# Seven block products for eight in the second phase's up product, two token tiles interleaved

## The chip, the cores and the metric

The kernel runs on one core of a Trainium2 chip. The metric is the device time of one execution in microseconds (us). Arithmetic is fp32 throughout: each fp32 operand of the large products is split into a high part, rounded to the type fp32r, and a low part, the remainder, and a product is three matmuls (high by high, high by low, low by high).

## The reference

Three layers follow each other: a retention layer with a decaying state (4 batches, 8 heads, 768 positions, head size 64), a feed-forward layer of 512 to 2048 to 512, and a second one of 512 to 1024 to 512. The last one is what the change touches. There are 3072 tokens.

```python
def _moe2_ref(x, w_in, w_out, g_ln):
    h = x @ w_in                                    # 3072 x 512 by 512 x 1024
    h_max = np.max(h, axis=-1, keepdims=True)
    e = np.exp(h - h_max)
    sm = e / (np.sum(e, axis=-1, keepdims=True) + 1e-09)
    solu = h * sm
    mu = np.mean(solu, axis=-1, keepdims=True)
    var = np.mean((solu - mu) ** 2, axis=-1, keepdims=True)
    ln = (solu - mu) / np.sqrt(var + 1e-06) * g_ln
    return (ln @ w_out).astype(np.float32)
```

## The kernel before

**Two phases.** The first phase computes retention and the first feed-forward layer in six blocks of 512 tokens and stores its result, transposed, to DRAM (x2T, stored by SP from the tile y). The second phase takes x2T in pairs of tiles of 128 tokens, 12 pairs and 24 tiles. Each engine has its own queue and runs it in program order; all order between engines is by semaphores written by hand.

**First phase, where it touches the change.** In each of 16 steps f of a block TensorE does `up(blk, f)` (12 matmuls of 512 columns) and `down(blk, f - 2)` (12 matmuls). VectorE clamps h (L610), ScalarE squares (L481), VectorE takes the maximum (L615), ScalarE copies the high part of g (L429), POOL subtracts for the low part (L670). In the last block `prepare(f)` of ScalarE and VectorE splits the second phase's w_in, its first two pairs of x2 and w_out between these steps, and POOL makes the low parts of w_out (L677). Its last two down products run behind the first up of the second phase. `evacuate`, which empties the accumulator banks to y for the last store of x2T, is called late, from the second phase's loops (ScalarE L429, VectorE L573). SP's queue holds the last four stores of x2T ahead of all its work of the second phase.

**Second phase.** `up(t)` is 24 matmuls: x's high and low parts are the stationary operand (128 x 128), w_in the moving one (512 columns), two banks of 512 columns for a tile, four of the eight banks for two tiles. VectorE searches the maximum over 1024 in PSUM (L866), ScalarE takes the exponential with its sum (L816), VectorE multiplies e, 1/sum and h from PSUM with the sum of the result (L878, "softening"), ScalarE squares with a sum (L821), POOL raises the variance to the power -0.5 (L924), VectorE normalises to z (L889) and transposes within squares of 32 (L893). SP stores z to DRAM and reads it back in four parts so that it comes back transposed. ScalarE copies its high part (L794) and VectorE subtracts for the low part (L861), in two halves. `down(t)` is 24 matmuls with z as the stationary operand into one of two banks; it waits for the output of two tiles ahead to be copied out (`o_ready`). ScalarE copies the result (`output`, L794) and SP stores it.

The order on TensorE is up 0, the last two downs of the first phase, up 1, up 2, and from then on up t with down t - 3 behind it, so a tile's z has some three tiles of TensorE's work to come back; the last downs follow without ups. The two split operations of x for a later pair (ScalarE L794, VectorE L853) stand ahead of the maximum of every other tile. A load of x2T for pair n waits for the end of up of pair n - 2.

Of the kernel before, what the change touches and what calls it, by code (L numbers as in the profile page):

```python
# [11 lines left out]
P = 128  # L12
# [8 lines left out]
KT = DM // P  # L21
# [35 lines left out]
def passes(a, b):  # L57
# [3 lines left out]
STATISTICS = ("h_max", "neg_max", "e_sum", "e_sum_eps", "e_inv", "s_sum", "neg_mean", "sq_sum", "var",  # L61
              "rstd")


def place(nc):
# [38 lines left out]
    split("x", [P, KT, BLK])  # L104
    plain("y", [P, KT, BLK])
# [23 lines left out]
    split_in_place("x2_0", [P, KT, 2 * P])  # L129
# [3 lines left out]
    split_in_place("x2_1", [P, KT, 2 * P])  # L133
    assert cursor[0] <= w_at + 5 * 8192
    for name in ("e", "solu", "dev", "z"):
        plain(name, [P, FF2])
    plain("o", [P, 2, DM])
    plain("zq", [P, 2, P // SQ, FT2, SQ])
    plain("zt", [P, 2, P // SQ, FT2, SQ])
    for n in range(LAG2):  # L140
        split(f"zT{n}", [P, FT2, P])
    assert cursor[0] <= w_at + 13 * 8192
# [3 lines left out]
def first_phase(nc, block, io, sem, mem, x2_dram, finish):  # L146
# [9 lines left out]
    with ExitStack() as ctx:  # L156
# [38 lines left out]
        def _(sp):  # L195
# [74 lines left out]
            for m in range(KT):  # L270
                sp.wait_ge(sem["x2_stored"][m], 16)
            x2_view = x2_dram.rearrange("(kt p) t -> p kt t", p=P)
            sp.dma_start(mem["x2_0_raw"][:, :, :], x2_view[:, :, 0:2 * P]).then_inc(sem["x2_loaded"][0], 16)
# [4 lines left out]
            sp.dma_start(mem["x2_1_raw"][:, :, :], x2_view[:, :, 2 * P:4 * P])\  # L278
                .then_inc(sem["x2_loaded"][1], 16)
# [147 lines left out]
        def _(act):  # L427
# [28 lines left out]
            def prepare(f):  # L456
                if 5 <= f < 5 + KT:
                    kt = f - 5
                    act.wait_ge(sem["w2_in_loaded"][kt], 16)
                    copy(mem["w2_in"][0][:, kt, :], mem["w2_in_raw"][:, kt, :]).then_inc(sem["w2_in_hi"], 1)  # L460
                elif f == 9:
                    act.wait_ge(sem["x2_loaded"][0], 16)
                    copy(mem["x2_0"][0][:, :, :], mem["x2_0_raw"][:, :, :]).then_inc(sem["x2_hi"], 1)
# [5 lines left out]
                elif f == 15:  # L469
                    act.wait_ge(sem["x2_loaded"][1], 16)  # L470
                    copy(mem["x2_1"][0][:, :, :], mem["x2_1_raw"][:, :, :]).then_inc(sem["x2_hi"], 1)
# [33 lines left out]
        def _(dve):  # L505
# [69 lines left out]
            def prepare(f):  # L575
                if 5 <= f < 5 + KT:
                    kt = f - 5
                    dve.wait_ge(sem["w2_in_hi"], kt + 1)
                    tt(mem["w2_in"][1][:, kt, :], mem["w2_in_raw"][:, kt, :],
                       mem["w2_in"][0][:, kt, :].bitcast(F32), ALU.subtract).then_inc(sem["w2_in_lo"], 1)  # L580
                elif f == 9:
                    dve.wait_ge(sem["x2_hi"], 1)
                    tt(mem["x2_0"][1][:, :, :], mem["x2_0_raw"][:, :, :],
                       mem["x2_0"][0][:, :, :].bitcast(F32), ALU.subtract).then_inc(sem["x2_lo"], 1)
# [8 lines left out]
                elif f == 15:  # L593
                    dve.wait_ge(sem["x2_hi"], 2)
                    tt(mem["x2_1"][1][:, :, :], mem["x2_1_raw"][:, :, :],
                       mem["x2_1"][0][:, :, :].bitcast(F32), ALU.subtract).then_inc(sem["x2_lo"], 1)
# [38 lines left out]
        def _(pool):  # L635
# [28 lines left out]
            def dense(blk):  # L664
                for f in range(FT1):
# [8 lines left out]
                    if blk == BLOCKS - 1 and 12 <= f < FT1:  # L674
                        for piece in (2 * (f - 12), 2 * (f - 12) + 1):
                            pool.wait_ge(sem["w2_out_hi"], piece + 1)
# [14 lines left out]
def second_phase(nc, block, io, sem, mem, x2_dram, z_dram, finish):  # L691

    TILES = TOKENS // P
    SEGS = [slice(n * 512, (n + 1) * 512) for n in range(FF2 // 512)]
    x2_view = x2_dram.rearrange("(kt p) t -> p kt t", p=P)
# [311 lines left out]
```

## Time and profile before

| | us |
|---|---|
| median of 3 runs | 880.04 (879.76 to 880.24) |
| the profiled execution, its time | 879.7 |
| its span, first to last instruction | 877.6 |
| TensorE busy | 871.1 (99%) |
| VectorE busy | 407.8 (46%) |
| ScalarE busy | 284.0 (32%) |
| POOL busy | 206.0 (23%) |

Busy time is the time in which an engine had an instruction in work. The page also cuts the span in 40 slices. TensorE's granted clock is full in all of them; in the 12 slices of the second phase VectorE is at 4 to 7 tenths, ScalarE at 2 to 4, and DMA engines at about 4 tenths. Matmuls overlap, so one of 512 columns has a duration of 0.39 us though they start every 0.227. A group of instructions is named by its line, engine, operation, and what it writes and reads.

### The profile page before, as it was taken

What the parts mean: (1) busy time and instruction counts of PE and PEld (TensorE: products, weight loads), DVE (VectorE), ACT (ScalarE), POOL (GpSimd) and SP (SyncE); (2) the same over time, 40 slices, a digit from 0 to 9 for tenths busy, and PEclk for the clock granted to TensorE, in tenths of its full rate; (3) what the DMA queues carried; (4) which work ended last, traced back from release to release, by engine and by line L of the source; (5) the groups of instructions that cost most, each with busy time, mean ns of one, the idle gap of its engine ahead of it and who ended that gap; (6) DMA issues with size and microseconds to landing.
All of it is one profiled execution on the core that took longest, in us unless ns stands there. A gap on an engine that the chain in (4) does not pass through costs nothing.

```text
span 877.6 us, 11925 instructions
## 1 busy us (share of the span) xinstructions
PE 871.1 (99%) x4888; PEld 712.7 (81%) x4888; DVE 407.8 (46%) x645; ACT 284.0 (32%) x454; POOL 206.0 (23%) x186
## 2 busy tenths in 40 slices
PE   8999999999999999999999999999999999999998
PEld 7788878888878888888878888888888888888886
DVE  5555443334332343323433332443666666666672
ACT  3333342212221132212321232334334444444442
POOL 2645532232223222232221122226000000000000
PEclk9999999999999999999999999999999999999999
DMA  9921111111111102111111004300444444444433
GB/s 338 375 68 49 49 49 49 49 52 46 61 49 49 57 28 96 49 49 37 49 37 49 25 1 167 121 1 1 144 133 156 156 144 144 144 155 147 150 125 132
DMA packets 50742, 82.85 MB, mean 94 GB/s; under 512 B 5248, under 2 KB 23680, under 8 KB 50688
## 3 DMA queue, kind: packets, MB, share of 16 engines
q1 hardware_dynamic: 50688, 82.08, 27.8%
q8 instruction: 39, 0.64, 0.3%
q14 instruction: 15, 0.12, 0.0%
HBM read 56.90 MB, written 25.17 MB: 94 GB/s over the span
## 4 chain that ended last, share of the span: by engine, by line
PE 94%; DVE 2%; DMA 2%; ACT 1%; POOL 1%; SPq 1%; issue 0%; DVEq 0%; POOLq 0%; ACTq 0%
PE acc L390 30%; PE h L360 29%; PE o_ps L778 14%; PE h L763 12%; PE att L297 2%; PE att L308 2%; PE att L332 1%; PE att L322 1%; DMA q<-in_q 1%; DMA x_raw<-x2T 0%; PE acc L308 0%; POOL w_out_lo L677 0%; DMA z<-zq 0%; PE h L377 0%; SPq L197 0%
## 5 line engine op out<-in xcount | busy, mean ns | idle before, releaser
L390 PE MATMUL acc<-g_hi,w 128*128 128x512 f32 x768 | 257.3, 396 | 0.0
L360 PE MATMUL h<-x_hi,w 128*128 128x512 f32 x760 | 250.0, 390 | 0.5 <-DVE x_lo L565 0.5
L670 POOL TENSOR_TENSOR g_lo<-g_raw,g_hi 128x512 fp32r<-128x512 f32 x96 | 123.4, 1286 | 399.7 <-ACT g_hi L429 399.7
L481 ACT ACTIVATE g_raw<-g_raw,half_bias 128x512 f32<-128x512 f32 x96 | 69.5, 724 | 337.9 <-DVE g_raw L610 337.9
L390 PEld LDWEIGHTS acc<-g_hi,w 128*128 128x128 f32 x768 | 144.2, 188 | 35.0 <-issue 3.4
L360 PEld LDWEIGHTS h<-x_hi,w 128*128 128x128 f32 x760 | 142.7, 188 | 30.6 <-DVE x_lo L565 0.9
L610 DVE TENSOR_SCALAR g_raw<-h 128x512 f32<-128x512 f32 x96 | 66.3, 691 | 180.7 <-PE acc L390 179.9
L390 PE MATMUL acc<-g_lo,w 128*128 128x512 f32 x384 | 149.7, 390 | 0.0
L360 PE MATMUL h<-x_lo,w 128*128 128x512 f32 x380 | 148.0, 389 | 0.0
L615 DVE TENSOR_TENSOR g_raw<-h,g_raw 128x512 f32<-128x512 f32 x96 | 66.4, 692 | 70.0 <-ACT g_raw L481 70.0
L429 ACT ACTIVATE g_hi<-g_raw 128x512 fp32r<-128x512 f32 x96 | 60.7, 632 | 72.7 <-DVE g_raw L615 72.7
L390 PEld LDWEIGHTS acc<-g_lo,w 128*128 128x128 f32 x384 | 72.2, 188 | 14.0
L360 PEld LDWEIGHTS h<-x_lo,w 128*128 128x128 f32 x380 | 71.4, 188 | 14.6
L763 PE MATMUL h<-w_in_hi,x_hi 128*128 128x512 f32 x192 | 74.8, 390 | 0.0
L763 PE MATMUL h<-w_in_lo,x_hi 128*128 128x512 f32 x192 | 74.7, 389 | 0.0
L778 PE MATMUL o_ps<-w_out_lo,zT_hi 128*128 128x512 f32 x192 | 74.7, 389 | 0.0
L763 PE MATMUL h<-w_in_hi,x_lo 128*128 128x512 f32 x192 | 74.7, 389 | 0.0
L778 PE MATMUL o_ps<-w_out_hi,zT_hi 128*128 128x512 f32 x192 | 74.7, 389 | 0.0
L778 PE MATMUL o_ps<-w_out_hi,zT_lo 128*128 128x512 f32 x192 | 74.7, 389 | 0.0
L924 POOL TENSOR_TENSOR rstd<-var,power 128x1 f32<-128x1 f32 x24 | 13.2, 548 | 227.5 <-DVE var L886 227.5
L816 ACT ACTIVATE e<-h,neg_max 128x1024 f32<-128x1024 f32 x24 | 26.8, 1117 | 86.7 <-DVE neg_max L868 86.6
L821 ACT ACTIVATE dev<-solu,neg_mean 128x1024 f32<-128x1024 f32 x24 | 27.7, 1153 | 46.8 <-DVE neg_mean L881 46.8
(76 smaller groups left out, 842.0 us busy)
## 6 DMA issues: line engine op xcount, KB each, us to landing
z<-zq SPq DMA_DIRECT2D x24, 512.0 KB, 2.7
zt<-z SPq DMA_DIRECT2D x96, 128.0 KB, 2.9
kT<-in_kT SPq DMA_DIRECT2D x24, 256.0 KB, 2.6
q<-in_q SPq DMA_DIRECT2D x24, 256.0 KB, 2.6
v<-in_v SPq DMA_DIRECT2D x24, 256.0 KB, 2.9
x2T<-y SPq DMA_DIRECT2D x24, 256.0 KB, 2.6
x_raw<-x2T SPq DMA_DIRECT2D x12, 512.0 KB, 4.3
out<-o SPq DMA_DIRECT2D x24, 256.0 KB, 2.1
```

Source lines behind the costliest of these rows:

```text
L297: last = mm(out[e][:, p * P:(p + 1) * P], kT[half(e), p, :], q[half(e), p, :], start=True, stop=True)
L360: last = mm(hb[f % 2][:, :], ww, xx[:, kt, :], start=kt == 0 and t == 0, stop=kt == KT - 1 and t == 2)
L390: last = mm(acc[m][:, :], ww, gg[:, f % 2, :], start=f == 0 and t == 0, stop=f == FT1 - 1 and t == 2)
L429: return nc.scalar.activation(out, in_, ACT.Copy)
L481: nc.scalar.activation(gate[:, f % 2, :], gate[:, f % 2, :], ACT.Square, bias=half_bias[:, 0:1], scale=0.5).then_inc(sem["squared"], 1)
L610: nc.vector.tensor_scalar(gate[:, f % 2, :], h, 1.0, -1.0, ALU.min, ALU.max)\
L615: tt(gate[:, f % 2, :], h, gate[:, f % 2, :], ALU.max).then_inc(sem["gmax"], 1)
L670: tt(g[1][:, f % 2, :], gate[:, f % 2, :], g[0][:, f % 2, :].bitcast(F32), ALU.subtract)\
L763: last = mm(hp[t % 2][:, seg], xx[:, kt, cols], ww[:, kt, seg], start=kt == 0 and i == 0, stop=kt == KT - 1 and i == 2)
L778: last = mm(op[t % 2][:, :], zz[:, f, :], ww[:, f, :], start=f == 0 and i == 0, stop=f == FT2 - 1 and i == 2)
L816: nc.scalar.activation(e[:, :], hp[t % 2][:, :], ACT.Exp, bias=st("neg_max", t), accum_out=st("e_sum", t)).then_inc(sem["e_ready"], 1)
L821: nc.scalar.activation(dev[:, :], solu[:, :], ACT.Square, bias=st("neg_mean", t), accum_out=st("sq_sum", t)).then_inc(sem["sq_sum"], 1)
```

## The change

The up product of a pair of tiles is a product of 256 x 512 by 512 x 1024. As 2 x 2 blocks by 2 x 2 blocks (token tile by half of the inner dimension; half of the inner dimension by half of the columns) it is done with seven block products for eight (Strassen's scheme in Winograd's form). A block product is 128 x 256 by 256 x 512, that is two steps by three passes, 6 matmuls. The sums that it needs are made once for w_in (VectorE, during the last block of the first phase, three sums of 128x1024, split in high and low parts as well) and for each pair for x (POOL, `sums_of_x2`: four operations over 256 elements, in a row through semaphores), and split by ScalarE and VectorE. VectorE's `join(n)` adds the block products together to h in SBUF, and four of its additions also give the maximum. The splits of the next pair stand within the join, from pair 1 on. All seven blocks pass through six banks (`pb`), of which for pair 0 only the first three or four are used, because the accumulators of the first phase still hold two others.

The two tiles of a pair then go side by side through maximum, exponential and so on, second tile first. z is made by ScalarE (`normalize`, an activation with rstd as scale and a bias) from a bias that VectorE computes. e and squares share a tile; h is read from SBUF. The downs go by slots s, two per pair. The order of TensorE is up 0, the last two downs of the first phase, up 1, down 0, up 2, down 1, down 2, up 3, down 3, down 4, and so on to up 9, down 15, down 16, up 10, down 17, up 11, downs 18 to 23.

The core of the diff:

```diff
@@ first phase, SP
+            for n in range(2):
+                sp.wait_ge(sem["g_used"], FT1 * (BLOCKS - 1) + 8 + 2 * n)
+                sp.dma_start(mem[f"x2_{n}_raw"][:, :, :], x2_view[:, :, n * 2 * P:(n + 1) * 2 * P])\
+                    .then_inc(sem["x2_loaded"][n], 16)
             store_x2(BLOCKS - 1)
@@ POOL
+            def sums_of_x2(n):
+                raw, out = mem[f"x2_{n % 2}_raw"], mem[f"x2_sum{n % 2}_raw"]
+                first, second = slice(0, P), slice(P, 2 * P)
+                pool.wait_ge(sem["x2_loaded"][n % 2], 16 * (n // 2 + 1))
+                tt(out[:, 0, :, :], raw[:, 0:2, second], raw[:, 2:4, second], ALU.add)\
+                    .then_inc(sem["x2_summed"], 1)
+                tt(out[:, 2, :, :], raw[:, 0:2, first], raw[:, 0:2, second], ALU.subtract)\
+                    .then_inc(sem["x2_summed"], 1)
...
@@ second phase, TensorE
-                for seg in SEGS:
-                    for kt in range(KT):
-                        for i, (xx, ww) in enumerate(passes(x[t // 2 % 2], w_in)):
-                            last = mm(hp[t % 2][:, seg], xx[:, kt, cols], ww[:, kt, seg],
-                                      start=kt == 0 and i == 0, stop=kt == KT - 1 and i == 2)
+                product(pb[0], a(0, FIRST), b(0, LEFT))
+                wait(pe, sem["h_max"], 2 * n)
+                product(pb[1], a(1, FIRST), b(1, LEFT))
+                if n == 0:
+                    pe.wait_ge(sem["gmax"], BLOCKS * FT1)
+                product(pb[2], s(1), t(1))
+                product(pb[3], s(2), b(0, RIGHT))
+                if n == 0:
+                    pe.wait_ge(sem["part_copied"], 1)
+                if n == 1:
+                    for par in range(2):
+                        pe.wait_ge(sem["acc_free"][par], 2 * BLOCKS)
+                product(bank4(n), a(1, SECOND), t(2))
+                pe.wait_ge(sem["taken"], 5 * n + 1)
+                product(bank5(n), s(0), t(0))
+                if n == 0:
+                    pe.wait_ge(sem["taken"], 2)
+                product(bank3(n), s(3), b(1, RIGHT))
...
+            for n in range(PAIRS2 - 1):
+                up(n)
+                if n == 0:
+                    finish["down"]()
+                if n >= 2:
+                    down(2 * n - 3)
+                if 1 <= n < PAIRS2 - 2:
+                    down(2 * n - 2)
+            up(PAIRS2 - 1)
+            for s in range(TILES - 6, TILES):
+                down(s)
@@ second phase, ScalarE
+            for n in range(PAIRS2):
+                copy_part(n)
+                if 1 <= n < PAIRS2 - 1:
+                    split_x(n + 1)
+                if n:
+                    split_z(2 * n - 2)
+                exponential(n, SECOND)
+                exponential(n, FIRST)
+                if n:
+                    split_z(2 * n - 1)
+                squares(n, SECOND)
+                squares(n, FIRST)
+                normalize(n, SECOND)
+                normalize(n, FIRST)
+                if n == 0:
                     finish["act_evacuate"]()
+                if 2 <= n < PAIRS2 - 1:
+                    output(2 * n - 3)
+                if 1 <= n < PAIRS2 - 2:
+                    output(2 * n - 2)
+            for s in range(TILES - 6, TILES - 4):
+                output(s)
@@ second phase, VectorE
+            def join(n):
+                dve.wait_ge(sem["part_copied"], n + 1)
+                dve.wait_ge(sem["products"], 7 * n + 2)
+                add_with_maximum(h2[:, FIRST, LEFT], pb[1][:, :], part[:, :], -3.4e38, st("h_first", FIRST))\
+                    .then_inc(sem["taken"], 1)
+                dve.wait_ge(sem["products"], 7 * n + 3)
+                tt(part[:, :], pb[2][:, :], part[:, :], ALU.add).then_inc(sem["taken"], 1)
+                if 1 <= n < PAIRS2 - 1:
+                    split_x(n + 1, False)
+                dve.wait_ge(sem["products"], 7 * n + 4)
+                dve.wait_ge(sem["taken"], 5 * n + 2)
+                tt(part7[:, :], pb[3][:, :], part[:, :], ALU.add).then_inc(sem["taken"], 1)
+                if 1 <= n < PAIRS2 - 1:
+                    split_x(n + 1, True)
...
+            for n in range(PAIRS2):
+                join(n)
+                if n:
+                    split_z(2 * n - 2)
+                soften(n, SECOND)
+                soften(n, FIRST)
+                if n:
+                    split_z(2 * n - 1)
+                if n == 0:
                     finish["dve_evacuate"]()
+                variance(n, SECOND)
+                variance(n, FIRST)
+                bias(n, SECOND)
+                bias(n, FIRST)
+                turn_squares(n, SECOND)
+                turn_squares(n, FIRST)
@@ second phase, SP
+            sp.wait_ge(sem["g_used"], BLOCKS * FT1)
+            for n in range(PAIRS2):
+                if n + 2 < PAIRS2:
+                    load_x2(n + 2)
+                if 2 <= n < PAIRS2 - 1:
+                    store(2 * n - 3)
+                put_z(2 * n)
+                put_z(2 * n + 1)
+                get_z(2 * n)
+                get_z(2 * n + 1)
+                if 1 <= n < PAIRS2 - 1:
+                    store(2 * n - 2)
```

## Rows read from the trace of the kernel before

**Rows 1.** The page, busy time of each engine and share of the span
```profile
PE 871.1 (99%) x4888; PEld 712.7 (81%) x4888; DVE 407.8 (46%) x645; ACT 284.0 (32%) x454; POOL 206.0 (23%) x186
```

**Rows 2.** Chain that ended last, in order of time: start, us, what
```profile
624.28 3.24 DMA z<-zq
...
629.47 4.11 DMA x_raw<-x2T
...
645.97 5.44 PE o_ps L778 x24
...
847.25 27.21 PE o_ps L778 x120
874.48 0.60 ACT o L794
```

**Rows 3.** Groups by line, 620 to 860 us: busy us, mean ns
```profile
L893 DVE STREAM_TRANSPOSE zq<-z 128x1024 f32<-128x1024 f32 x24 | 29.9, 1246 | 0.8
L878 DVE SCALAR_TENSOR_TENSOR solu<-e,e_inv,h 128x1024 f32<-128x1024 f32 x23 | 29.4, 1280 | 0.8
L861 DVE TENSOR_TENSOR zT_lo<-zt,zT_hi 128x512 fp32r<-128x512 f32 x45 | 28.3, 667 | 1.8 <-ACT zT_hi L794 1.8
L866 DVE TENSOR_REDUCE h_max<-h 128x1 f32<-128x1024 f32 x23 | 28.0, 1216 | 0.0
...
L816 ACT ACTIVATE e<-h,neg_max 128x1024 f32<-128x1024 f32 x23 | 25.7, 1117 | 81.3 <-DVE neg_max L868 81.2
L889 DVE TENSOR_SCALAR z<-solu,neg_mean,rstd 128x1024 f32<-128x1024 f32 x24 | 19.5, 813 | 16.0 <-POOL rstd L924 16.0
...
L853 DVE TENSOR_TENSOR x_lo<-x_raw,x_hi 128x1024 fp32r<-128x1024 f32 x10 | 12.2, 1220 | 0.9 <-ACT x_hi L794 0.9
L794 ACT ACTIVATE o<-o_ps 128x512 f32<-128x512 f32 x20 | 11.5, 577 | 0.0
```

**Rows 4.** Timeline of VectorE at the transition: start, us, operation, idle before
```profile
609.14 0.69 DVE L615 TENSOR_TENSOR g_raw<-h,g_raw 128x512 f32<-128x512 f32 x1 [0.79 <-ACT g_raw L481]
611.48 1.47 DVE L595 TENSOR_TENSOR x_lo<-x_raw,x_hi 128x1024 fp32r<-128x1024 f32 x1 [1.65 <-ACT x_hi L429]
615.41 1.23 DVE L866 TENSOR_REDUCE h_max<-h 128x1 f32<-128x1024 f32 x1 [2.46 <-POOL power L920]
```

**Rows 5.** Timeline of all engines, 742 to 747 us, a tile's statistics
```profile
742.71 0.15 DVE L873 TENSOR_SCALAR e_sum_eps<-e_sum 128x1 f32<-128x1 f32 x1 [1.27 <-ACT e L816]
...
744.60 1.15 ACT L821 ACTIVATE dev<-solu,neg_mean 128x1024 f32<-128x1024 f32 x1 [1.93 <-DVE neg_mean L881]
...
745.88 0.15 DVE L886 TENSOR_SCALAR var<-sq_sum 128x1 f32<-128x1 f32 x1 [1.31 <-ACT dev L821]
...
746.69 0.81 DVE L889 TENSOR_SCALAR z<-solu,neg_mean,rstd 128x1024 f32<-128x1024 f32 x1 [0.66 <-POOL rstd L924]
```

**Rows 6.** Timeline of POOL, two subtractions of 512 elements each
```profile
600.95 2.54 POOL L677 TENSOR_TENSOR w_out_lo<-w_out_raw,w_out_hi 128x512 fp32r<-128x512 f32 x2
...
611.83 3.51 POOL L677 TENSOR_TENSOR w_out_lo<-w_out_raw,w_out_hi 128x512 fp32r<-128x512 f32 x2
```

**Rows 7.** Timeline of SP's queue at the transition
```profile
621.75 1.79 SPq L222 DMA_DIRECT2D x2T<-y  x4
...
627.54 1.75 SPq L731 DMA_DIRECT2D zt<-z  x4
```

**Rows 8.** The page, DMA issues: count, KB each, us to landing
```profile
z<-zq SPq DMA_DIRECT2D x24, 512.0 KB, 2.7
```

**Rows 9.** Timeline of ScalarE, the first z that comes back
```profile
631.95 1.15 ACT L794 ACTIVATE zT_hi<-zt 128x512 fp32r<-128x512 f32 x2 [1.99 <-DMA zt<-z]
```

**Rows 10.** Timeline of TensorE at the start of the kernel
```profile
1.19 2.93 PE L411 MATMUL acc<-warm 128*128 128x256 f32 x6 [1.19 <-DVE warm L621]
...
7.29 1.56 PE L411 MATMUL acc<-warm 128*128 128x256 f32 x6
```

**Rows 11.** Windows: busy of five engines, granted clock, DMA share, GB/s
```profile
0.00:5.00 5.00, 3.74 (x18) 2.69 (x20) 0.28 (x2) 1.49 (x2) 0.20 (x4) 1.00 0.59 200
```

More of the change, by code:

```diff
@@ L141, in place @@
         split(f"zT{n}", [P, FT2, P])
-    assert cursor[0] <= w_at + 13 * 8192
+    assert cursor[0] <= y_at
+    cursor[0] = y_at
+    plain("o", [P, 2, DM])
     return mem
@@ L742, in _ @@
+            for n in range(PAIRS2):
[9 more added lines that the diff above has]
+                    store(2 * n - 2)
+            for s in range(TILES - 5, TILES):
+                store(s)
             for par in range(2):
@@ L747, in _, with product, up, a @@
             mm = nc.tensor.matmul
-            def up(t):
-                if t == 0:
+            def product(out, a, b):
+                for k in range(2):
+                    for i, (aa, bb) in enumerate(passes([part(k) for part in a], [part(k) for part in b])):
+                        last = mm(out[:, :], aa, bb, start=k == 0 and i == 0, stop=k == 1 and i == 2)
+                last.then_inc(sem["products"], 1)
+            def up(n):
+                def a(half_k, tile):
+                    return [lambda k, x=x: x[:, 2 * half_k + k, tile * P:(tile + 1) * P]
+                            for x in mem[f"x2_{n % 2}"]]
+                def s(i):
+                    return [lambda k, x=x: x[:, i, k, :] for x in mem[f"x2_sum{n % 2}"]]
+                def b(half_k, cols):
+                    return [lambda k, w=w: w[:, 2 * half_k + k, cols] for w in w_in]
+                def t(i):
+                    return [lambda k, w=w: w[:, i, k, :] for w in w_sum]
+                if n == 0:
                     pe.wait_ge(sem["probs"], 2 * CHUNKS)
@@ L803, in split_z @@
+            def split_z(s):
+                act.wait_ge(sem["zt_loaded"][s % 2], 64 * (s // 2 + 1))
+                wait(act, sem["o_done"], s - LAG2 + 1)
                 for n in range(2):
                     fs = slice(4 * n, 4 * n + 4)
[L805 to L811 removed]
@@ L838, in _, with output @@
-            split_z(TILES - 3)
-            squares(TILES - 1)
-            output(TILES - 5)
+                    copy(zT[s % LAG2][0][:, fs, :].rearrange("p f (i c) -> p f i c", c=SQ),
+                         zt[:, s % 2, :, fs, :].rearrange("p i f c -> p f i c")).then_inc(sem["zT_hi"], 1)
+            def output(s):
+                act.wait_ge(sem["o_done"], s + 1)
+                wait(act, sem["o_stored"][s % 2], 16 * (s // 2))
+                if s == 0:
+                    for m in range(KT):
+                        act.wait_ge(sem["x2_stored"][m], 16 * BLOCKS)
+                copy(o[:, s % 2, :], op[s % 2][:, :]).then_inc(sem["o_ready"], 1)
@@ L843, in _ @@
             split_z(TILES - 1)
-            for t in range(TILES - 3, TILES):
-                output(t)
+            for s in range(TILES - 3, TILES):
+                output(s)
         @block.vector
```

404 lines of the change are left out of this document (222 added, 182 removed).

## The prediction

> **What bounds the kernel now.** I read the page's busy line first: TensorE is busy for 871.1 us of a span of 877.6 [rows 1], so only its work and its gaps count. Next the chain that ended last, in order of time: in the second phase it is groups of 24 matmuls of 5.44 us one behind the other, a tile's up product or its down product, so 0.2267 us a matmul, and the last of them ends at 874.48, 3.1 us ahead of the end [rows 2]. There is no pause that a shorter stream could move into. The other engines have room: the groups by line give what each operation costs [rows 3]. The change takes matmuls away and lengthens the chain from an up product to the z that the down product needs. The question is whether that chain, so far three tiles ahead of TensorE, stays hidden.
>
> **What goes.** A pair of tiles took 48 up matmuls and takes 7 x 6 = 42. Twelve pairs save 72 x 0.2267 = 16.3 us if TensorE never waits. Bound: no row shows another pace for this shape, so 16.3 is the whole gain.
>
> **What the other engines do for a pair, and the steady state.** VectorE loses two searches for the maximum (1.216) and two z (0.813) and gets, per pair, three additions from PSUM (0.69, [rows 4]), four additions with a maximum, and one more split of 128x1024 (1.22). The addition with a maximum is in no row; it lies between the plain PSUM addition, 0.69, and the softening operation over 1024, 1.28 [rows 3]; I take 0.75, nearest to the same shape with one small accumulator read more. Join: 4 x 0.75 + 3 x 0.69 + 2 x 1.22 + 0.3 = 7.8. The rest: z splits 2.5, softening 2 x 1.85, four small statistics 0.6, two transposes 2.5. Waits that remain: the variance to what uses rstd is 0.81 for one tile, from 745.88 to 746.69 [rows 5] and POOL and ScalarE in front of the first transpose add as much again, together 1.6. Sum 18.7 us. TensorE has 42 + 48 = 90 matmuls, 20.4 us, per pair. So VectorE goes from loosely used to 92%, yet TensorE still bounds. ScalarE gets two normalisations of 128x1024 (the nearest rows are the exponential, 1.12, and the square, 1.15 [rows 3, 5]; 1.1 taken), a copy of 0.58 and a split near 1.1; it has about 12.5 of 20.4. The new POOL sums are four operations of 256 elements. A POOL subtraction of 512 elements took 1.27 alone and 3.51 for two beside VectorE [rows 6]; in proportion 0.65 for 256, at most 1.3; I take 0.7, 2.8 per pair, off the path in the steady state. The z round trip of one pair (softening to z back in SBUF) is 18 to 19 us, and the down product wants it 25.8 us behind the end of its up product. Price of the steady state: 0.
>
> **End of the first phase.** The extra splits give VectorE at most 1 us more than an iteration's 5.44 in three iterations running, and its results lead TensorE by 3; nothing, at most 0.5.
>
> **Transition, first places.** The up product of pair 0 uses only four banks, so its sixth block waits for VectorE's first addition. VectorE waits for POOL's constant behind w_out pieces, as now: its first operation of the phase starts at 615.41 [rows 4]. Plus 0.75, the sixth block starts at 616.2; without waits it would be at 614.2, and a copy behind ScalarE's splits has used 0.2 of that. Cost 2.05. Up ends at 619.0, the two remaining down products of the first phase end at 624.4, the first four blocks of pair 1 at 629.85. The fifth block needs the accumulator banks evacuated. ScalarE does that now behind normalisation. In the trace's time: second tile's negative maximum 619.9, first tile's 620.8; exponentials, for which VectorE waits 1.27 [rows 5]; two softenings of 1.85 each, from the first small statistic at 742.71 to ScalarE's square at 744.60 [rows 5], end at 624.95; squares and variance 626.3; rstd for both and bias 627.65; normalisations to 629.4; evacuation 630.0 and 630.5. The fifth block waits 0.7. Up 1 ends at 634.65.
>
> **Transition, the long pause.** Down 0 follows here, where it used to come behind four tiles' ups. Several things now stand in series. SP's queue holds the four stores of x2T (0.45 each, [rows 7]) ahead of all else of the second phase; they wait for the late evacuation, so they end at 631.85. Behind them SP issues the load of pair 2. A load of this kind took 4.11 and a z store beside x2T stores 3.24 where 2.7 is usual [rows 2, 8]; I take 4.4: 636.25. POOL's sums wait for it: 639.0. VectorE stands inside the join of pair 1, after its second addition, since both splits of pair 2 wait for the sums. Queued behind that wait are two splits, one plain addition, the sums of the other blocks and the maxima, 2.44 + 2.25 + 1.4 + 0.3 = 6.4 to 645.4, and only then the low half of z, 0.67 for its first half: 646.2 with the passing of semaphores. z itself is back earlier: its store goes behind the load at 632.2, 3.3 later the four reads, 4.4 later [rows 7, 9] 639.9. TensorE waits from 634.65 to 646.2, 11.55. Bounds: if the additions run end to end and the sums take 0.65, 2 less; if the sums take 1.3 each, 2.4 more.
>
> **TensorE after the pause.** At the start, its first six matmuls of 256 columns took 2.93 us and the same six later 1.56, with a granted clock of 1.00 (2.4 GHz) in the row of that stretch [rows 10, 11]. So a start from idle has cost 1.37 here. I add 1.4 for the 11.5 us pause, between 0 and twice that. TensorE: Matmul & The Clock Gate, section Part 1 of the Trainium skill, says that an idle TensorE falls to 1.2 GHz and returns once busy. The matmul durations agree with it, the granted clock of the row does not; by the granted clock alone the forecast would be 1.4 lower.
>
> **The end.** Only one down product stands between up 10 and up 11, and the output of down 18 is queued on ScalarE behind the whole last pair. Count from the end of up 10: first exponential 0.95; softenings end 6.75, z halves 7.95, bias 8.8, normalised 10.1, transposed 11.4. SP has the store of output 17 in front: z store at 12.2, reads at 14.9, z back at 19.3. ScalarE is in order, so the exponential of pair 11 starts behind z's high half at 20.5 although its maximum is long there; normalised twice at 29.9, output 18 at 30.5. Down 20 wants that bank at 5.44 + 9.52 + 10.88 = 25.84. Cost 4.7. Then four downs and the same last 3.1 us.
>
> **Sum.** -16.3 + 2.05 + 0.7 + 11.55 + 1.4 + 4.7 = +4.1. The profiled execution of 879.7 (span 877.6, 2.1 around it) becomes 883.8. It lies 0.34 under the median 880.04 of the runs, so the forecast is 884.1.
>
> **Rivals.**
> *The low bounds hold together*: additions and sums 2 less, the load 0.3, no cost behind the pause 1.4, the end 1. That is 4.7 less, 879.4, within what can be told from none. For it: neighbours without a wait overlap by some 0.08 in the trace. Against: most steps here wait for the one before. Chance 0.17.
> *Faster*: the pause ends when z is back, not with the sums. It decides at whether pair 2's load leaves SP before about 627; then down 0 starts at 640.5, 5.7 earlier, and with no cost behind a shorter pause 1.4 more goes: 877.0. The order of SP's queue in the diff speaks against it, and that the evacuation stands behind the normalisations. Chance 0.12.
> *The softening slows.* It read PSUM and SBUF at 1.28 [rows 3]; now both inputs are in SBUF. The splits also read two SBUF tensors and take 1.22 for 1024, which speaks against a slower pace, but they write no accumulator. At half the pace it is 1.07 more each: 2.1 in the transition, twice 2.1 at the end, and VectorE's loop of 18.7 becomes 20.8, 0.4 over TensorE's, some 1 to 2 in total: 892. Chance 0.13. Vector Engine (DVE) Microarchitecture Reference, Points that are easy to get wrong, in the Trainium skill, says that this operation with two sources in SBUF that aren't bf16 halves its throughput. By that, 892 is the forecast; no row of the trace has that form.
> *POOL and VectorE hold each other up.* A split took 1.47 beside POOL [rows 4] and 1.22 otherwise, POOL 3.51 for two. If the sums fall on the transposes and splits, 0.25 to 1 per pair comes on a loop with 1.7 to spare; with the transition's own splits and pieces, 3 more in all: 887. Chance 0.13.
>
> **How the numbers follow.** The forecast with its own bounds (881.8 to 887) has 0.45. Faster by over 0.2% (below 878.3) is the second rival, 0.12; within 0.2%, about what a measurement of this kernel can tell from no change, is the first, 0.17; slower is the rest, 0.71. The range takes in the faster rival and the halved softening: 877 to 892.5.
>
> **What would show it.** Right: no waits of TensorE between up 3 and up 9; one pause of 10 to 13 us in front of the first down product, released by VectorE's low half of z; SP's x2T stores near 630 and the pair's load behind them; a second pause near 4.7 in front of the down product of slot 20, released by ScalarE's output. 72 matmuls fewer at 0.2267. Softening at 1.28. Wrong: a pause below 8 us, a wait of TensorE in each pair, a softening near 2.3, or an addition with maximum above 1.0.

## The result

| | us |
|---|---|
| before, median of 6 runs | 880.14 (879.76 to 882.25) |
| changed, median of 6 runs | 888.6 (886.47 to 891.81) |
| ratio changed to before | 1.0098, 95% interval 1.0076 to 1.0119 |
| profiled execution of the changed kernel, its time and span | 891.81, 890.0 |

The change makes the kernel 8.5 us slower. The forecast was 4.1 slower. The profiled execution is the longest of the six, 3.2 us over the median, which matters when its rows are added up below.

The page of the changed kernel, the line that answers to [rows 1], and its line of TensorE's granted clock in 40 slices:

```profile
PE 864.4 (97%) x4816; PEld 704.5 (79%) x4816; DVE 447.4 (50%) x772; ACT 333.1 (37%) x505; POOL 242.5 (27%) x234
...
PEclk9999999999999999999999999999979999999989
```

TensorE has 6.7 us less busy time than before where 16.3 of work went, and of the 40 slices one shows a granted clock of 7 tenths and one of 8, all others 9 or more. The chain that ended last, in order of time (start, us, what), answers to [rows 2]:

```profile
618.86 4.56 PE p L842 x12
623.42 5.48 PE acc L401 x24
...
650.85 8.28 PE o_ps L895 x24
659.14 9.52 PE p L842 x42
668.66 10.88 PE o_ps L895 x48
...
862.01 24.86 PE o_ps L895 x96
886.90 0.60 ACT o L914
```

In the steady state an up of a pair is 42 matmuls in 9.52 us and two downs are 10.88, with no wait between them from 659.14 until the sixth block of the last pair at 844. But 12 matmuls of the up of pair 0 took 4.56 where 2.72 is the pace, the 24 of the first down 8.28 instead of 5.44, and the last 96 took 24.86 instead of 21.76. The timeline of TensorE has the waits in front of them (start, us, operation, idle before and what ended it), here the sixth block of pair 0's up:

```profile
618.86 0.79 PE L842 MATMUL p<-w_sum_hi,x_sum_hi 128*128 128x512 f32 x1 [2.19 <-DVE h_first L993]
```

the first down:

```profile
650.85 0.79 PE L895 MATMUL o_ps<-w_out_hi,zT_hi 128*128 128x512 f32 x1 [11.93 <-DVE zT_lo L1077]
```

and the down of slot 20:

```profile
862.01 0.80 PE L895 MATMUL o_ps<-w_out_hi,zT_hi 128*128 128x512 f32 x1 [3.72 <-ACT o L914]
```

And the windows of these stretches (busy of five engines, then granted clock, DMA share, GB/s):

```profile
618.86:622.00 3.14, 3.14 (x7) 2.48 (x8) 2.11 (x5) 0.00 (x0) 1.80 (x2) 0.50 0.00 0
638.90:650.80 11.90, 0.02 (x1) 0.00 (x0) 6.50 (x14) 4.86 (x7) 2.85 (x4) 0.66 0.80 252
650.80:656.00 5.20, 5.15 (x12) 4.08 (x13) 4.99 (x13) 4.07 (x7) 0.00 (x0) 0.50 0.00 0
862.00:868.00 6.00, 5.99 (x14) 4.75 (x15) 0.76 (x1) 0.44 (x1) 0.00 (x0) 0.50 0.77 279
```

After each of the three longer pauses the granted clock is 0.50, that is 1.2 GHz, for 3.3, 5.4 and 6.0 us, and matmuls of 512 columns start every 0.43 us (618.86 to 622.0 holds seven).

**The account of this execution**, from start times of matmuls less 0.2267 for the one before: TensorE stood still for 0.52 (ahead of the up of pair 0), 2.34, 0.36, 12.09, 0.46 (sixth block of the last pair) and 3.88 us, 19.65 in all. The slow stretches cost 1.68 + 2.68 + 2.93 = 7.29. The second phase was reached 1.72 later than in the trace of before. In the first 20 us of this execution the granted clock was 0.91, with 0.50 from 7.8 to 11.2 us. The 1.72 belongs to the execution and not to the change: the same point of the first phase comes 0.55 later than in before in e4's profiled execution, and 3.2 later in e6's. -16.32 + 19.65 + 7.29 + 1.72 = 12.34; measured between the last matmuls' ends (886.90 and 874.48) 12.42.

### The profile page after: what moved, and what is told of

The parts are those of the page before. It is cut to its first block, busy times and chain, and to the rows that moved or that the text cites. A ratio compares the mean times of both kernels' runs of the same rounds, so it can differ in the third digit from the quotient of the medians.

```text
span 890.0 us, 12101 instructions
## 1 busy us (share of the span) xinstructions
PE 864.4 (97%) x4816; PEld 704.5 (79%) x4816; DVE 447.4 (50%) x772; ACT 333.1 (37%) x505; POOL 242.5 (27%) x234
## 4 chain that ended last, share of the span: by engine, by line
PE 90%; DVE 3%; DMA 2%; POOL 2%; issue 1%; ACT 1%; SPq 0%; DVEq 0%; ACTq 0%; POOLq 0%
PE acc L401 30%; PE h L371 28%; PE o_ps L895 14%; PE p L842 10%; PE att L308 3%; PE att L319 2%; PE att L343 1%; PE att L333 1%; POOL w_out_lo L720 1%; DVE solu L1047 1%; DMA q<-in_q 1%; DVE h L993 1%; DMA x_raw<-x2T 1%; DVE zT_lo L1077 0%; ACT solu L941 0%
## 5 line engine op out<-in xcount | busy, mean ns | idle before, releaser
L895 PE MATMUL o_ps<-w_out_hi,zT_hi 128*128 128x512 f32 x192 | 77.3, 403 | 15.7 <-DVE zT_lo L1077 11.9
L895 PE MATMUL o_ps<-w_out_lo,zT_hi 128*128 128x512 f32 x192 | 76.8, 400 | 0.0
L895 PE MATMUL o_ps<-w_out_hi,zT_lo 128*128 128x512 f32 x192 | 76.6, 399 | 0.0
L895 PEld LDWEIGHTS o_ps<-w_out_hi,zT_hi 128*128 128x128 f32 x192 | 37.4, 195 | 24.3 <-DVE zT_lo L1077 12.4
L914 ACT ACTIVATE zT_hi<-zt 128x512 fp32r<-128x512 f32 x48 | 27.5, 620 | 56.4 <-DMA zt<-z 56.4
L895 PEld LDWEIGHTS o_ps<-w_out_hi,zT_lo 128*128 128x128 f32 x192 | 37.3, 194 | 8.1
L895 PEld LDWEIGHTS o_ps<-w_out_lo,zT_hi 128*128 128x128 f32 x192 | 37.4, 195 | 7.9
L532 DVE TENSOR_TENSOR pr<-att,mask 128x512 f32<-128x512 f32 x40 | 25.7, 685 | 25.2 <-PE att L308 25.2
```

Source lines behind the costliest of these rows:

```text
L532: tt(of("pr", c)[:, e, :, :], by_pair(s_banks(c)[e]), mask[:, e, :, :], ALU.mult)\
L895: last = mm(op[s % 2][:, :], zz[:, f, :], ww[:, f, :], start=f == 0 and i == 0, stop=f == FT2 - 1 and i == 2)
L914: return nc.scalar.activation(out, in_, ACT.Copy)
```

## The experiments

All were run beside the kernel before, whose medians in the three groups of runs were 880.49, 880.09 and 880.62. Theory A is mostly the forecast's chain, with TensorE's clock added as what it under-counted. The changed kernel was not run again beside them, so the gains below are against its 888.6, whose own six runs spread over 5.3 us. Its ratio's interval, 1.0076 to 1.0119, overlaps those of e3, e5 and e9 and touches e1's: by time alone these four gains are not clear of noise, and what they show is in their traces. Gains and losses of the others are clear.

| run | edit to the changed kernel | median us | ratio to before, 95% |
|---|---|---|---|
| e1_fill | unread matmuls in two pauses | 885.45 | 1.0064 (1.0052 to 1.0076) |
| e2_load_first | load of pair 2 ahead of x2T stores | 883.41 | 1.0033 (1.0020 to 1.0046) |
| e3_pool_last | w_out pieces 4, 5 behind the constant | 886.37 | 1.0069 (1.0057 to 1.0082) |
| e4_output | output 18 ahead of the last squares | 883.65 | 1.0039 (1.0027 to 1.0051) |
| e5_evac | evacuation ahead of normalisations | 887.66 | 1.0082 (1.0068 to 1.0096) |
| e6_three | e2, e3 and e4 | 876.72 | 0.9957 (0.9944 to 0.9971) |
| e7_filled | e6, z store first, output 20 earlier, fill | 874.52 | 0.9940 (0.9925 to 0.9955) |
| e8_double | first block product twice | 900.99 | 1.0236 (1.0222 to 1.0250) |
| e9_pool_clear | POOL's pieces behind the splits | 886.49 | 1.0070 (1.0057 to 1.0082) |
| e10_best | e7 with e9's edit and x2T stores behind z's reads | 872.32 | 0.9907 (0.9892 to 0.9923) |

### e1_fill: is it the clock?

```diff
+                if s == 0:
+                    pe.wait_ge(sem["w2_out_lo"], 1)
+                    fill(op[1], 50)
+                if s == TILES - 4:
+                    pe.wait_ge(sem["h_max"], 2 * PAIRS2)
+                    fill(pb[0], 16)
                 wait(pe, sem["o_ready"], s - 1)
```

> Edit: 50 matmuls of 512 columns whose results nobody reads are put ahead of the first down product, and 16 ahead of the down product of slot 20, so that TensorE works through most of its two long pauses (12.0 and 3.9 us); the waits stay. Theory A (what the forecast missed is the clock after a pause): the rows after both pauses show a granted clock of 0.50 for 5.4 and 6.0 us; with the fill they show 1.00, the 24 matmuls of the first down take 5.4 instead of 8.1 us and the last four downs 21.8 instead of 24.9; time falls by about 5.6 us to some 883. Theory B (the excess is lateness of the chain through VectorE, DMA and ScalarE, and the slow matmuls only move into a gap that is there anyway): time within 1 us of the changed kernel's 888.6.

Windows of e1 behind both filled pauses:

```profile
649.00:656.00 7.00, 6.45 (x29) 5.29 (x29) 6.10 (x17) 5.04 (x11) 0.93 (x2) 1.00 0.01 2
857.00:863.00 6.00, 5.82 (x26) 4.47 (x25) 2.08 (x2) 1.76 (x3) 0.00 (x0) 1.00 0.58 223
```

The clock stayed at 1.00 behind both, and the first down took 5.74 and the last four 22.11 in the chain. The waits are still there, filled. The time fell by 3.15 us, not by 5.6: the expectation was made from the profiled execution, whose clock was lower than that of the others (mean granted clock over the span 0.985, against 0.987 to 0.992). What is left of e1, 5.0 over before, is almost what the sum makes without the clock behind the two filled pauses: -16.3 + 19.7 + 1.7, the last for the slow matmuls behind the pause of 2.3 us, which is not filled. So theory A holds for the cause. The 3.15 us may be less than what the two pauses cost in clock: all five executions of e1 have a mean granted clock of 0.998, which is what one fall behind the pause of 2.3 us makes in the profiled one, while e2, e4 and e5 had no fall there. If the changed kernel's median execution had none either, the fill took away up to 3.15 + 1.7 = 4.9 us, an estimate; no such execution was profiled.

### e2_load_first: what makes the long pause?

```diff
-            store_x2(BLOCKS - 1)
+            finish["store_x2"] = lambda: store_x2(BLOCKS - 1)
...
+            load_x2(2)
+            finish["store_x2"]()
             sp.wait_ge(sem["g_used"], BLOCKS * FT1)
             for n in range(PAIRS2):
-                if n + 2 < PAIRS2:
+                if 1 <= n and n + 2 < PAIRS2:
                     load_x2(n + 2)
```

> Edit: SP issues the load of pair 2 of x2T ahead of the last four stores of x2T instead of behind them. Theory A (the long pause is the chain late evacuation, stores, load, sums, join): the load leaves near 623.5 instead of 636.1, the sums are done by 631, the join of pair 1 ends some 6 us earlier, near 644, and what ends the pause is then z, which came back at 646.5; the pause shrinks from 12.1 to about 8.5, time falls by 3 to 4 us. Theory B (z's way through DRAM ends the pause and the load is hidden beside it): less than 1 us.

The way from the load to the first down in the changed kernel, first SP's queue:

```profile
634.01 1.81 SPq L232 DMA_DIRECT2D x2T<-y  x4
636.06 0.37 SPq L797 DMA_DIRECT2D x_raw<-x2T  x1
636.49 1.28 SPq L807 DMA_DIRECT2D z<-zq  x2
642.16 3.65 SPq L815 DMA_DIRECT2D zt<-z  x8
```

POOL's first and last sum:

```profile
640.92 0.72 POOL L728 TENSOR_TENSOR x_sum_raw<-x_raw 128x256 f32<-128x256 f32 x1 [9.49 <-DMA x_raw<-x2T]
...
643.21 0.72 POOL L736 TENSOR_TENSOR x_sum_raw<-x_raw,x_sum_raw 128x256 f32<-128x256 f32 x1
```

VectorE's split that waits for them, and the low half of z at the end:

```profile
644.03 1.23 DVE L999 TENSOR_TENSOR x_lo<-x_raw,x_hi 128x1024 fp32r<-128x1024 f32 x1 [7.74 <-POOL x_sum_raw L736]
...
650.12 1.28 DVE L1077 TENSOR_TENSOR zT_lo<-zt,zT_hi 128x512 fp32r<-128x512 f32 x2
```

and ScalarE's high half of z:

```profile
646.48 1.15 ACT L914 ACTIVATE zT_hi<-zt 128x512 fp32r<-128x512 f32 x2 [1.46 <-DMA zt<-z]
```

The order is as the forecast had it: stores until 635.8, load, 4.8 us later the sums, and VectorE idle for 7.74 us in the middle of the join. z was back at 646.5 and waited until 650.1. With the load ahead (e2), SP's queue:

```profile
621.21 0.36 SPq L797 DMA_DIRECT2D x_raw<-x2T  x1
631.90 1.79 SPq L232 DMA_DIRECT2D x2T<-y  x4
633.80 1.18 SPq L807 DMA_DIRECT2D z<-zq  x2
```

and TensorE's first down in e2:

```profile
643.14 0.80 PE L897 MATMUL o_ps<-w_out_hi,zT_hi 128*128 128x512 f32 x1 [6.34 <-DVE zT_lo L1079]
```

The pause went from 12.09 to 6.49 us and the time fell by 5.2 us, more than the 3 to 4 expected: the join was over at 640.2, and z was back at 641.7. That is 4.8 earlier than in the changed kernel's trace, but 2.1 of it is that TensorE came to the pause 2.1 earlier in this execution, at 636.65 instead of 638.76, mostly because the clock did not fall behind the pause of 2.3 us. From z's store to its use it is 7.9 us where it was 10.0. Theory B falls. z's way is the bound once the load is out of it.

### e3_pool_last and e4_output: the first and the last pause

```diff
-                        for piece in {12: (0, 1), 14: (2, 3), 15: (4, 5)}.get(f, ()):
+                        for piece in {12: (0, 1), 14: (2, 3)}.get(f, ()):
...
             pool.wait_ge(sem["power_set"], 1)
+            finish["pool_w2_out"](4)
+            finish["pool_w2_out"](5)
             finish["pool_w2_out"](6)
```

> Edit: POOL makes w_out's low pieces 4 and 5 behind its setting of the constant instead of ahead, so VectorE's first addition no longer waits for them. Theory A: the addition starts near 616.5 instead of 618.1, the sixth block of pair 0 waits under 0.7 us instead of 2.3, and TensorE keeps its full clock, so that the twelve matmuls behind it take 2.7 instead of 4.4 us; all later work of the chain moves 2 to 3 us forward and the time falls by 3 us or more. Theory B (the clock falls at any pause, and the evacuation's path decides the rest): the pause shrinks but the clock still falls, time falls by under 1 us.

The first addition started at 616.89 and the sixth block's wait shrank to 1.06 us; its twelve matmuls ran at full clock. 2.2 us less, under the expected 3. VectorE's split of the sums, still 2.31 us long, was now what it waited for; e9 takes that up. All waits of TensorE together fell by only 1.0, from 19.65 to 18.68, since the fifth block's and the long one grew a little. That the clock stayed up behind this wait is not shown to be the edit's doing, since in e2, e4 and e5 it also stayed up behind the unchanged 2.3 us.

```diff
                 if n:
                     split_z(2 * n - 1)
+                if n == PAIRS2 - 1:
+                    output(TILES - 6)
                 squares(n, SECOND)
...
-            for s in range(TILES - 6, TILES - 4):
-                output(s)
+            output(TILES - 5)
```

> Edit: ScalarE copies the output of slot 18 out ahead of the squares of the last pair instead of behind its normalisations. Theory A (the last pause is ScalarE's queue): the down product of slot 20 starts without a wait and at full clock; the wait moves to slot 22, whose z comes back near 870, about 2 us late, so 3.9 + 2.9 go and some 2 come back: 4 to 5 us less. Theory B (z of the last pair is the bound anyway and the pause only moves): under 1 us less.

The last pause of e4:

```profile
867.09 0.50 PE L895 MATMUL o_ps<-w_out_hi,zT_hi 128*128 128x512 f32 x1 [1.47 <-ACT o L914]
```

5.0 us less, as theory A has it: the wait of 3.88 us ahead of slot 20 is gone, one of 1.63 stands ahead of slot 22, and the clock did not fall behind it. It is ended by ScalarE's copy of output 20, which was queued behind z's split. The shorter wait makes 2.25 of the 5.0 and leaves 2.75 for the clock, near the 2.93 that the slow matmuls behind this pause cost in the changed kernel's profiled execution. e1 gained 3.15 from two pauses together. The two runs agree only if the changed kernel's median execution, unlike e1's, had no fall of the clock behind the first pause; that is not shown.

### e5_evac: a gain given back by the transfers

```diff
                 squares(n, FIRST)
+                if n == 0:
+                    finish["act_evacuate"]()
                 normalize(n, SECOND)
                 normalize(n, FIRST)
-                if n == 0:
-                    finish["act_evacuate"]()
```

> Edit: ScalarE evacuates its two accumulator banks ahead of the two normalisations of pair 0 instead of behind them; z of pair 0 comes about 1 us later for it. Theory A (the late evacuation holds the stores, the load and with it the join): stores and load leave 2.4 us earlier, the fifth block of pair 1 no longer waits, the long pause ends about 2.3 us earlier; time falls by 2 to 2.5 us. Theory B (z's own way is the bound at the long pause): the pause ends no earlier or 1 us later, time unchanged or up by 1.

In e5 SP's queue:

```profile
628.89 1.80 SPq L232 DMA_DIRECT2D x2T<-y  x4
630.93 0.37 SPq L797 DMA_DIRECT2D x_raw<-x2T  x1
631.82 1.46 SPq L807 DMA_DIRECT2D z<-zq  x2
```

and ScalarE's split behind the load:

```profile
637.14 1.06 ACT L914 ACTIVATE x_hi<-x_raw 128x1024 fp32r<-128x1024 f32 x1 [5.02 <-DMA x_raw<-x2T]
```

Neither holds in full: 0.9 us less, within what the runs' intervals can tell from none. The evacuation and the load moved as expected, the fifth block did not wait, and the pause fell to 10.69. But the load took 6.2 us from issue to ScalarE instead of 4.8. The order on SP's queue doesn't explain it: in the changed kernel the four stores of x2T ended as closely ahead of the load (0.2 us), and z's stores followed it sooner, within 0.43 us instead of 0.9. The cause of the longer load stays open.

### e6_three and e8_double: do the parts add up?

> Edit: the three reorderings of e2, e3 and e4 together, the same work on every engine as in the changed kernel. Theory A (each removes its own pause): gaps of TensorE of some 0.5 + 1.1 + 0.5 + 6.5 + 0.5 + 1.6 = 10.7 us remain, 880.5 - 16.3 + 10.7 = 874.9, with a clock loss of up to 1 behind the longest; the sum of the separate gains gives 875.7. Theory B (the pauses are one chain and each gain is given back at the next): 879 or more.

876.72: 3.4 us faster than before, 11.9 less than the changed kernel, where the separate gains of e2, e3 and e4 make 5.2 + 2.2 + 5.0 = 12.4. TensorE's gaps in it are 0.52, 1.05, 0.50, 6.50, 0.47 and 1.73, 10.8 us against 10.7 expected, and the slow matmuls of the first down cost 2.3 more: -16.3 + 10.8 + 2.3 is -3.2, measured is -3.4. The pauses are separate terms and not one chain.

```diff
                 pe.wait_ge(sem["x2_lo"], 2 * n + 2)
+                for k in range(2):
+                    for i, (aa, bb) in enumerate(passes([q(k) for q in a(0, FIRST)], [q(k) for q in b(0, LEFT)])):
+                        mm(pb[0][:, :], aa, bb, start=k == 0 and i == 0, stop=k == 1 and i == 2)
```

> Edit: the changed kernel, with the first block product of every pair done twice, so that each pair again has 48 up matmuls; results as before. Theory A (the seven-for-eight saving is won in full wherever TensorE bounds, and lost where a pause follows anyway): pairs 0, 1 and 11 run into their pauses, nine pairs cost 1.36 us each, 12.2 us more, some 901. Theory B (the steady state is bound by VectorE or by z's round trip, TensorE's work there is partly free): less than 6 us more, and waits of TensorE in each pair of the changed kernel's steady state.

12.4 us more than the changed kernel against 12.2. The saving of 1.36 us a pair is won whole in nine pairs; in three most of it is spent on waits: in e8 the pauses are 1.00, 11.25 and 3.33 where they were 2.34, 12.09 and 3.88, and the small waits of 0.36 and 0.46 are gone, 3.55 of the 4.08 us.

### e9_pool_clear: VectorE and POOL

```diff
-                        for piece in {12: (0, 1), 14: (2, 3), 15: (4, 5)}.get(f, ()):
+                        for piece in {12: (0, 1)}.get(f, ()):
...
-            finish["pool_w2_out"](6)
-            finish["pool_w2_out"](7)
+            pool.wait_ge(sem["x2_lo"], 4)
+            for piece in range(2, FT2):
+                finish["pool_w2_out"](piece)
```

> Edit: POOL makes w_out's low pieces 2 to 7 only when VectorE has split both pairs of x2 and their sums; before, they ran at the same time. Theory A (VectorE's operations with two inputs in SBUF and POOL's hold each other up): the splits of the sums take 1.22 instead of 2.32 us, the up of pair 0 starts without its 0.5 us wait, the first addition starts near 615.8, the sixth block waits under 0.3 us instead of 2.3, the clock does not fall there; 3.5 to 4.5 us less than the changed kernel. Theory B (2.32 is what this split costs, for another reason, and POOL only happens to be beside it): the split stays above 2 us, and the time falls by the 2 us that e3 gave.

In the changed kernel, VectorE's split of pair 1's sums:

```profile
614.61 2.31 DVE L633 TENSOR_TENSOR x_sum_lo<-x_sum_raw,x_sum_hi 128x1024 fp32r<-128x1024 f32 x1
```

and the pieces of w_out that POOL made beside and behind it:

```profile
613.56 4.47 POOL L720 TENSOR_TENSOR w_out_lo<-w_out_raw,w_out_hi 128x512 fp32r<-128x512 f32 x2
...
618.15 2.51 POOL L720 TENSOR_TENSOR w_out_lo<-w_out_raw,w_out_hi 128x512 fp32r<-128x512 f32 x2
```

In e9 the same split and the two softenings behind it:

```profile
612.70 1.21 DVE L633 TENSOR_TENSOR x_sum_lo<-x_sum_raw,x_sum_hi 128x1024 fp32r<-128x1024 f32 x1
...
620.03 1.42 DVE L1047 SCALAR_TENSOR_TENSOR solu<-e,e_inv,h 128x1024 f32<-128x1024 f32 x1
...
621.95 1.74 DVE L1047 SCALAR_TENSOR_TENSOR solu<-e,e_inv,h 128x1024 f32<-128x1024 f32 x1
```

and POOL's six pieces:

```profile
614.04 8.56 POOL L720 TENSOR_TENSOR w_out_lo<-w_out_raw,w_out_hi 128x512 fp32r<-128x512 f32 x6 [2.31 <-issue]
```

The split takes 1.21 us without POOL's work beside it and 2.31 with it. Two pieces took POOL 4.47 beside the splits and 2.51 behind them. Theory A holds for the mechanism: the 2.34 us wait is gone and the clock did not fall there. The wait of 2.34 had two parts, though: POOL's constant, which also came behind the pieces, and the long split; e3 alone had removed the first and left 1.06. Theory A fails for the size, 2.1 us less instead of 3.5 to 4.5. The 0.51 ahead of the up of pair 0 stayed, since that split still met POOL's low part of g, and the pieces now met the softenings, which read two SBUF tensors in this kernel and took 1.42 and 1.74 instead of 1.28; the fifth block then waited 1.13 and the long pause was 12.42. SBUF — State Buffer, section Who interferes with whom, in the Trainium skill, states this rule: a VectorE instruction with two inputs in SBUF and a GpSimd instruction that reads SBUF take turns on one port, whole instructions at a time. These rows agree.

### e7_filled and e10_best: what is left of the long pause

e7 is e6 with the stores of x2T behind z's store, output 20 ahead of the last but one split of z, and a fill of 18 ahead of the first down:

```diff
                 put_z(2 * n + 1)
+                if n == 0:
+                    finish["store_x2"]()
                 get_z(2 * n)
                 get_z(2 * n + 1)
...
             output(TILES - 5)
+            output(TILES - 4)
             split_z(TILES - 2)
-            output(TILES - 4)
```

> Edit: e6 and three more: SP stores z of pair 0 ahead of the last x2T stores, ScalarE copies output 20 out ahead of the last but one split of z, and 18 matmuls that nobody reads stand ahead of the first down product. Theory A: z of pair 0 is back 1.8 us earlier, so the long pause is near 4.7 us of which 4.1 are filled, the clock stays full, the last wait is 0.5 shorter: 872 to 873. Theory B (the x2T stores only take the DMA engines from z's reads): no better than e6.

e10 is e7 with e9's edit in place of e3's, a fill of 20, and the x2T stores behind the reads of z:

```diff
                 put_z(2 * n + 1)
-                if n == 0:
-                    finish["store_x2"]()
                 get_z(2 * n)
                 get_z(2 * n + 1)
+                if n == 0:
+                    finish["store_x2"]()
```

> Edit: e9 with the load of pair 2 ahead, ScalarE's outputs of slots 18 and 20 ahead as in e7, the x2T stores behind the reads of pair 0's z instead of between its store and its reads, and 20 matmuls that nobody reads ahead of the first down product. Theory A (z's way through DRAM, held up by the x2T stores, ends what is left of the long pause): z is back 8 us after its store instead of 10.2, against e7 2.2 from that, 1.5 from the first places, 1 to 2 of clock and pause: 869 to 870.5. Theory B (z's way has its length whatever runs beside it): 872 to 873.

SP's queue in e7:

```profile
630.35 1.40 SPq L807 DMA_DIRECT2D z<-zq  x2
631.79 2.85 SPq L232 DMA_DIRECT2D x2T<-y  x4
634.69 4.18 SPq L815 DMA_DIRECT2D zt<-z  x8
```

ScalarE's first half of z in e7:

```profile
640.54 1.15 ACT L927 ACTIVATE zT_hi<-zt 128x512 fp32r<-128x512 f32 x2 [7.09 <-DMA zt<-z]
```

SP's queue in e10:

```profile
630.15 1.41 SPq L807 DMA_DIRECT2D z<-zq  x2
632.80 3.67 SPq L815 DMA_DIRECT2D zt<-z  x8
636.51 2.02 SPq L232 DMA_DIRECT2D x2T<-y  x4
```

and ScalarE's first half of z in e10:

```profile
637.25 1.15 ACT L927 ACTIVATE zT_hi<-zt 128x512 fp32r<-128x512 f32 x2 [3.99 <-DMA zt<-z]
```

With the x2T stores between z's store and its reads, z is back 10.2 us after its store; with the stores behind the reads, 7.1; with the stores ahead of z's store, as in e2 and e6, it was 7.9. So e7's expectation was wrong there, its pause 6.6 (18 filled matmuls, 4.08, and 2.53 unfilled) and not 4.7, and the pauses sum to 10.67, as e6's 10.77. The gain of 2.2 over e6 is in no wait and goes with the clock: two of e7's five executions had a mean granted clock of 1.000 (873.4 and 873.9), none of e6's did (0.995 or 0.996). In e7's profiled execution it still fell, behind the unfilled 2.53 us. In e10 the wait ahead of the first down is covered by the fill of 20, no stretch behind a wait runs at half clock, and the gaps left are 0.52, 1.08, 0.46 and 1.33. e10 is the version that beats both: 872.32, 8.3 us under before and 16.3 under the changed kernel. The sum 880.62 - 16.32 + 4.53 for the fill + 3.39 for the gaps gives 872.22. The time is 1.8 to 3.3 us over the expected 869 to 870.5, and 1.08 of that is the fifth block's wait for the evacuation, which was not counted. It lies in theory B's 872 to 873, but B's mechanism falls by the rows, 10.2 us against 7.1 for z's way; A's sum was too low. Its windows:

```profile
612.00:640.00 28.00, 27.08 (x119) 21.90 (x119) 24.59 (x51) 15.55 (x23) 13.72 (x14) 1.00 0.38 117
640.00:850.00 210.00, 209.70 (x926) 173.31 (x925) 168.67 (x366) 132.69 (x199) 37.75 (x58) 1.00 0.48 152
850.00:871.00 21.00, 16.45 (x72) 13.01 (x70) 2.59 (x4) 4.50 (x8) 0.00 (x0) 1.00 0.43 135
```

## Why the prediction was wrong

The direction, the steps and their places were right. The size was wrong by a factor of two, and most of it lies in one term: 3.75 of the 4.4 us that are missing.

**What goes** was right: 42 matmuls in 9.52 us, 72 x 0.2267.

**The steady state costs nothing**: right. The period of a pair is 20.40 us, with no wait of TensorE from pair 3 to pair 9. The groups by line of the steady stretch, 655 to 860, with mean ns, answer to [rows 3]:

```profile
L1047 DVE SCALAR_TENSOR_TENSOR solu<-e,e_inv,h 128x1024 f32<-128x1024 f32 x20 | 25.7, 1284 | 0.7
...
L993 DVE CUSTOM_DVE_ANT_0 h<-p,part,h_first 128x512 f32<-128x512 f32 x20 | 15.0, 751 | 2.7 <-DVE part L1029 0.4
L993 DVE CUSTOM_DVE_ANT_0 h<-p,part 128x512 f32<-128x512 f32 x20 | 13.7, 687 | 15.8 <-PE p L842 15.7
```

```profile
L941 ACT ACTIVATE solu<-solu,z_bias,rstd 128x1024 f32<-128x1024 f32 x21 | 25.0, 1238 | 9.3 <-DVE z_bias L1061 9.3
```

The addition with a maximum took 0.69 or 0.75 (0.75 taken). The softening with both inputs in SBUF took 1.284 against 1.280 before, so the rival of its halving is out. Vector Engine (DVE) Microarchitecture Reference, Points that are easy to get wrong, in the Trainium skill, says that this operation with two sources in SBUF that aren't bf16 halves its throughput. These rows don't show it, and the measurement decides. ScalarE's normalisation took 1.24, not 1.1.

**First phase and first places**: 0.52 + 2.34 + 0.36 = 3.2 where 2.05 + 0.7 was put. VectorE's first addition came at 618.11, 2.7 later than the forecast's 615.41. 1.7 of this is the later start of the second phase in this execution; the other 1.0 is POOL's two pieces ahead of its constant, which took 4.47 where they had taken 3.51 [rows 6]. That such pieces stretch beside VectorE's splits was known to the forecast, which made a rival of it and kept it out of the sum. The 0.52 ahead of the up of pair 0, behind the long split of the sums, was no term of it.

**The long pause**: 12.09 against 11.55, ended by VectorE's low half of z, as said. z's own way was put too short: back 5.3 us behind TensorE's stop in the forecast (639.9 and 634.65), 7.7 in the trace (646.5 and 638.8), which was hidden under the join.

**The end**: 3.88 against 4.7, plus 0.46 ahead of the sixth block of the last pair. The output of slot 18 was out at 862.0, where the forecast's clock of the last pair puts 862.4.

These make 19.65 against 19.0. **The failed step is the term TensorE after the pause**, 1.4 us for one pause. In the profiled execution it is 7.29 us for three pauses, and in the median one about 5: 8.5 + 16.3 - 19.65 = 5.15, of which e1's fill takes 3.15 away. Two things were mis-sized in it. The price of one fall came from the start of the kernel, where six short matmuls saw it [rows 10]; behind a pause in the full stream it was 1.7 to 2.9 us here, 1.5 to 3.0 over all runs. And the pauses of 2.3 and 3.9 us were given none, though nothing in the trace of before said that a shorter pause is free. That the windows row showed a full granted clock at the start [rows 11] had made the term look small; the same column shows 0.50 behind the pauses. At the very start the column is no evidence: e6's profiled execution has 1.00 there from 0 to 13.8 us, while its two groups of six short matmuls, at 1.18 and at 9.47, both took 2.93.

The two low rivals, the pause that ends with z and the low bounds together, are out by the same rows. The rival of POOL and VectorE had its mechanism right, at the transition only: 1.0 us on POOL's pieces and 1.1 on each split of the sums (2.31 against 1.21), not a cost in each pair.

## What to carry to other kernels

When TensorE bounds a kernel without a gap, work taken from it is a full gain only where the chain that feeds it has slack, so lay out the first and the last round as well as the steady one: here 9 of 12 pairs gained whole, and the pauses of the first two pairs and the last, 19.65 us, took more than all twelve had brought. Price each pause of TensorE twice, once for its length and once for the matmuls at half clock behind it; matmuls that nobody reads, put ahead of the wait, removed the second part where they left 0.7 us or less of it unfilled (e1, e10), and not in e7's profiled execution, where 2.5 were left. Look at what an in-order queue holds: three reorderings, one each of SP's, POOL's and ScalarE's queue, with no operation changed, turned 8.5 us of loss into 3.4 of gain (e6).

## What the runs showed of the hardware

- Behind a pause of 2.34 us TensorE's granted clock fell to 0.50 in two of the five profiled executions that had this pause (the changed kernel and e1; not in e2, e4 and e5). Behind the unfilled pauses of 3.3 to 4.0 and of over 6 us it fell each time. In e7 it also fell behind 18 unread matmuls and 2.53 us without any. It did not behind pauses of 1.0 to 1.7 us, nor behind any wait of e10. The slow stretch cost from 1.5 to 3.0 us. The changed kernel's runs spread over 5.3 us, the shortest (886.47) with a mean granted clock of 0.992 and the longest (891.81) with 0.985; e10's spread over 0.8 at 0.999 and 1.000.
- A split of 128x1024 with two SBUF inputs took 1.21 us alone and 2.32 beside POOL's subtraction, a softening 1.28 and 1.74, two POOL pieces 2.51 and 4.47.
- z's round trip through DRAM took 7.1 us, 7.9 with four stores of 256 KB issued ahead of its store (e2, e6), and 10.2 with them between its store and its reads (e7).
